# A gated recurrence and an expert layer in three-pass FP32: tokens per step from 512 to 468

## The reference

```python
# x, f_logit: (2, 6080, 256); w_in: (256, 2048); w_out: (2048, 256)
sig = 1 / (1 + exp(-f_logit))
f = lower_bound + (1 - lower_bound) * sig
i = 1 - f
for t in range(6080):
    h = f[:, t] * h + i[:, t] * x[:, t]     # one state per batch and channel
    y[:, t] = h
h = y.reshape(12160, 256) @ w_in
g = h * clip(h + 3, 0, 6) / 6
out = g @ w_out
```

## Time and profile before

| | |
|---|---|
| median of 3 runs | 1085.32 us (1084.63 to 1086.12) |
| span of the profiled execution, first to last instruction | 1083.2 us |
| around the span (median of the runs less the span) | 2.1 us |
| TensorE matmuls busy | 99% of the span, 4636 matmuls |
| VectorE / ScalarE / GpSimd busy | 57% / 49% / 7% |
| mean granted TensorE clock | 0.998 of full |
| memory traffic | 41.7 MB, 39 GB/s |

### The profile page before, as it was taken

The page is one execution under the profiler, slowest core; times in us unless marked ns, Lnnn a source line. Parts: engine busy times, 40 slices in busy tenths (PEclk is TensorE's granted clock), DMA queues, the critical chain, the costliest instruction groups (busy, mean ns, idle before and its releaser), DMA issues.

```text
span 1083.2 us, 12791 instructions
## 1 busy us (share of the span) xinstructions
PE 1074.5 (99%) x4636; PEld 873.8 (81%) x4636; DVE 621.4 (57%) x950; ACT 533.2 (49%) x859; POOL 70.9 (7%) x37
## 2 busy tenths in 40 slices
PE   7999999999999999999999999999999999999998
PEld 7998888888888888888888888888888888888886
DVE  7865564655646556465564655646556465564644
ACT  5655454454544545444454444544445445454443
POOL 3300000000000000000000000000000000000000
PEclk9999999999999999999999999999999999999999
DMA  7011010110101101011010110101101001010000
GB/s 262 1 56 56 1 59 0 58 58 0 58 6 52 58 0 58 13 46 58 0 58 17 41 58 0 58 21 37 58 0 58 24 34 58 0 58 20 1 20 19
DMA packets 22093, 41.74 MB, mean 39 GB/s; under 512 B 1600, under 2 KB 3136, under 8 KB 22080
## 3 DMA queue, kind: packets, MB, share of 16 engines
q1 hardware_dynamic: 22080, 41.56, 11.4%
HBM read 29.10 MB, written 12.45 MB: 38 GB/s over the span
## 4 chain that ended last, share of the span: by engine, by line
PE 98%; DVE 0%; ACT 0%; issue 0%; ACTq 0%
PE y_ps L465 49%; PE h_ps L445 49%; DVE state L349 0%; DVE state_lo L379 0%; ACT clipped L263 0%; DVE g_lo L364 0%; DVE g L359 0%; DVE drive L342 0%; ACT y_sb L324 0%; ACT state_hi L277 0%; ACT g_hi L268 0%; ACTq L262 0%
## 5 line engine op out<-in xcount | busy, mean ns | idle before, releaser
L263 ACT ACTIVATE clipped<-h_ps,half 128x512 f32<-128x512 f32 (+1 forms) x384 | 263.2, 686 | 533.6 <-PE h_ps L445 533.6
L359 DVE SCALAR_TENSOR_TENSOR g<-clipped,h_ps 128x512 f32<-128x512 f32 (+1 forms) x384 | 261.7, 682 | 450.2 <-ACT clipped L263 450.1
L445 PE MATMUL h_ps<-state_hi,w_in_hi 128*128 128x512 f32 (+1 forms) x768 | 303.2, 395 | 3.3 <-DVE state_lo L379 3.3
L465 PE MATMUL y_ps<-g_hi,w_out_hi 128*128 128x512 f32 (+1 forms) x768 | 302.5, 394 | 1.0 <-DVE g_lo L364 1.0
L445 PE MATMUL h_ps<-state_lo,w_in_hi 128*128 128x512 f32 (+1 forms) x768 | 302.8, 394 | 0.0
L445 PE MATMUL h_ps<-state_hi,w_in_lo 128*128 128x512 f32 (+1 forms) x768 | 302.7, 394 | 0.0
L465 PE MATMUL y_ps<-g_lo,w_out_hi 128*128 128x512 f32 (+1 forms) x768 | 302.3, 394 | 0.0
L465 PE MATMUL y_ps<-g_hi,w_out_lo 128*128 128x512 f32 (+1 forms) x768 | 302.3, 394 | 0.0
L364 DVE TENSOR_TENSOR g_lo<-g,g_hi 128x512 fp32r<-128x512 f32 (+1 forms) x384 | 271.2, 706 | 0.2
L268 ACT CAST g_hi<-g 128x512 fp32r<-128x512 f32 (+1 forms) x384 | 233.0, 607 | 1.6 <-DVE g L359 1.4
L445 PEld LDWEIGHTS h_ps<-state_hi,w_in_hi 128*128 128x128 f32 x768 | 144.9, 189 | 37.0 <-DVE state_lo L379 2.9
(11 more groups left out here) (23 smaller groups left out, 77.9 us busy)
## 6 DMA issues: line engine op xcount, KB each, us to landing
z_sb<-in_z SPq DMA_DIRECT2D x22, 512.0 KB, 4.5
x_sb<-in_x SPq DMA_DIRECT2D x22, 512.0 KB, 5.1
out_y<-y_sb SPq DMA_DIRECT2D x21, 512.0 KB, 3.3
w_in_raw<-in_w_in SPq DMA_DIRECT2D x8, 256.0 KB, 5.9
w_out_raw<-in_w_out SPq DMA_DIRECT2D x8, 256.0 KB, 7.1
out_y<-y_sb SPq DMA_DIRECT2D x2, 448.0 KB, 3.5
out_y<-y_sb SPq DMA_DIRECT2D x2, 256.0 KB, 2.1
z_sb<-in_z SPq DMA_DIRECT2D x2, 224.0 KB, 3.7
```

What stands on the lines that cost most here:

```text
L263: nc.scalar.activation(clipped[:, s, 0:n], h_ps[:, s, 0:n], ACT.Relu, bias=half[:], scale=1.0 / 6.0).then_inc(clipped_ready, 1)
L359: nc.vector.scalar_tensor_tensor(g[:, s, 0:n], clipped[:, s, 0:n], 1.0, h_ps[:, s, 0:n], ALU.min, ALU.mult).then_inc(g_ready, 1)
L445: last = nc.tensor.matmul(h_ps[:, s, 0:n], w[:, f, k, :], v[:, b, k, 0:n], start=(k == 0 and m == 0), stop=(k == K - 1 and m == len(terms) ...
L465: last = nc.tensor.matmul(y_ps[:, b, d, 0:n], w[:, f, at], v[:, s, 0:n], start=(f == 0 and m == 0), stop=(f == F - 1 and m == len(terms) - 1))
```

## The change

A step covers N = 468 tokens rather than 512. By the same formulas there are 13 steps (STEPS), the first of N_FIRST = 6080 - 12 x 468 = 464 tokens, and 26 tiles. Every tensor in SBUF with N in its shape gets rows of 468 elements (1872 bytes) rather than 512 (2048 bytes); the PSUM tensors keep rows of 512, one bank. The last copy on VectorE gets its range written out, since `y_ps` rows are now longer than N.

```diff
-N = 512
+N = 468
...
-            nc.vector.tensor_copy(y_sb[:, B - 1, 0], y_ps[:, B - 1, 0]).then_inc(y_head_copied, 1)
+            nc.vector.tensor_copy(y_sb[:, B - 1, 0, 0:N], y_ps[:, B - 1, 0, 0:N]).then_inc(y_head_copied, 1)
```

## The result

The changed kernel takes 1079.07 us (1078.64 to 1079.21, 4 runs) against 1085.14 us (1084.63 to 1086.12, 4 runs): ratio 0.9939, 95% interval 0.9926 to 0.9951. It is faster by 0.6%, 6.1 us. 15.3 us (1.4%) were forecast: the direction was right, and the gain is 40% of the forecast one.

The account below looks back on a forecast made before the run. The prediction took TensorE's matmul stream to bound the kernel: 18.1 start-up + 75.1 + 970.9 stream + 3.3 tail + 0.5 remainder = 1067.9 us of span, plus 2.1 around it, 1070.0 us; range 1057 to 1097.

Parts of the forecast that it names:

- What bounds the kernel, the counts, the other engines: Whole span: TensorE's matmul distance sets the time; 4608 and 360 matmuls after start-up; the other engines' work stays hidden.
- Start-up and tail: Before the first `down` matmul, 17.8 us growing by 0.3 to 18.1; after the last matmul, 3.3 us unchanged.
- the remainder of 0.5 us: Part of the earlier kernel's span that its account left unexplained (1082.7 against 1083.2), kept in the forecast sum.
- The time around the span: Measured time outside the profiled span, put at 2.1 us and added to 1067.9 us.
- The disputed price: Start-to-start distance of the new matmuls: 210.7 ns for 468 columns, 208.6 for 464, a stream of 1046.0 us.
- the point of decision: Distance of 213.8 ns a matmul, from which the stream has no more room for a gain.
- a distance outside 208 to 216 ns: Sign in the middle of the run that would make the step from the two sizes wrong.
- its last rival: Rows of 1872 bytes or an engine falling behind: up to 234.3 ns for each matmul, time 1188; chance 0.05.
- the line: Distance of the stream's matmuls interpolated between 448 and 512 columns: 15.6 us less stream, time 1070.0; chance 0.30.
- The flat addition: Stream matmuls keep 13.3 ns on top of the columns up to 468, rising only nearer 512: time 1058.4; chance 0.27.
- The snap to 213.3 ns: Both new sizes' distance goes to 16 units of 13.33 ns: time 1083.8, no change; chance 0.13, shared with near-decision cases.
- The fixed 21 ns: Each matmul pays 21 ns on top of its columns, 448 columns being the exception: time 1096.5, slower; chance 0.25.

Follow-up runs that it names:

- alone: Kernel cut down to TensorE stretches of 96 matmuls, recurrence and expert layer left out; 512 columns took 226.7 ns at shift 0, 234.3 at 40.
- ten different beginnings: TensorE-only stretches of 448 columns (rows of 448, shift 40), all but the first after one matmul of another size; all ten had 200.0 ns.
- the first sweep: TensorE-only kernel, 20 stretches of 96 matmuls of varied column counts, rows of 512 elements: 226.7 ns at 512 columns, 211.8 at 468, 202.6 at 448.

## Why the prediction was wrong

**What bounds the kernel, the counts, the other engines.** Right. TensorE is 98% of the chain, there are 4608 and 360 matmuls, no wait in the middle, slack 3.0 us as worked out, VectorE 59%, the loop's further turn and the further transfers cost nothing.

**Start-up and tail.** 18.1 was forecast and 17.6 measured; 3.3 and 3.3; the remainder of 0.5 us was not there. Together 1.0 us less. The trace before shows where the remainder was: the first 132 matmuls of the stream, from 17.80 to 44.64 us, took 0.44 us more than at 200.0 ns each. The time around the span was 1.9 us and not 2.1.

**The disputed price.** This step failed: "I take the straight line between the two rows", 210.7 ns for 468 columns and 208.6 for 464, with nothing for the new row length. Measured were 212.8 and 210.5: 4608 x 2.08 = 9.6 us and 360 x 1.9 = 0.7 us too little. Less the 1.0 and 0.2 us above, that is the miss of 9.1 us. Its direction held, since 212.8 lies below the point of decision, 213.8. The sign that was to show a wrong step here, "a distance outside 208 to 216 ns", was too wide to show it.

The fault was to take the distance for a function of the number of columns. The additions of 21.0 ns at 512 and 13.3 at 448 belong to the one place that both had in the kernel before. The same 512 columns have 13.3 ns when the states and g are moved by 352 bytes (1053.74 us), and the same 448 have 20.0 ns in a kernel of 448 tokens, even at their old place. What the runs show is a cost that depends on where the moving operand starts against the weights, in the main modulo 256 bytes, together with the size and, at 468 columns, with the steady pattern that the stream falls into.

**The row length.** The change also took the rows from 2048 to 1872 bytes. The prediction had this in its last rival, with a chance of 0.05, the price of 512 columns, and "No row speaks for it". The mechanism was there and its size was wrong: 2.8 ns a matmul, 12.2 us, not 118. Its ground was wrong as well: starts "at multiples of 2048 bytes", which the expectation for rows of 512 elements repeats, were starts 2048 bytes apart but 160 bytes off the weights' place. With rows kept at 512 elements the change gives 1066.91 us and 210.0 ns, near the line's 1070.0 and 210.7, so the missing gain went there: 2.8 ns more by the rows, 0.7 less than the line without them. That the line was near in this case is luck: the 464 columns took 212.2 ns there and not 208.6, and at the other place, 352 bytes on, the line's end points and its sign are different.

**The rivals.** The flat addition did not come: 13.3 ns was no floor for 468 columns in any run (15.0 was the least). The snap to 213.3 ns was near to what came, with 212.8, and its time of 1083.8 is 4.7 us too much; but alone, 468 columns do sit at 210.0, 211.7 or 213.3 by place and start. The fixed 21 ns was wrong in its premise, as shown by the kernel with 512 tokens at 13.3.

**Open.** Why the difference of the places counts is not shown. That the reads of the weights and of the moving operand get in each other's way would fit the 512 columns (both moved: no cost; bfloat16: 2.5 ns), but it is argued, and it does not by itself account for the other sizes: 448 columns are cheaper at 40 (200.0 ns) than at 0 (202.6), and 384, 496 and 504 have the same distance at both. The Trainium skill, "TensorE: Matmul & The Clock Gate", section "Part 2: What happens when you issue a matmul", says that loading the next weights takes nothing from the running matmul's reads. For FP32R the place of the weights does change the distance, 226.7 against 234.3 ns with nothing else changed; whether the reads are what it changes, no run here shows. Open is also whether the row length or the places behind it make the 2.8 ns, and why 448 columns have 206.7 ns in the whole kernel and 200.0 alone; ten different beginnings did not bring 206.7 about.

## What to carry to other kernels

When matmuls set the time, read the distance of their starts and subtract columns / 2.4; if what is left differs between stretches, ask about places in memory as well as sizes. A line through two sizes of one trace holds, if at all, for the addresses of that trace: before it is used for a change that moves them, one size should be measured at other addresses. A tensor's row length and whatever is allocated ahead of it belong to the change, though no instruction shows them; 352 unused bytes were worth 31 to 32 us here, five times what the change brought.

## What the runs showed of the hardware

- FP32R matmuls with a weight load each, back to back at the granted clock of 1.00 (2.4 GHz): 13.3 ns on top of the columns at 256 and 512 columns when moving operand and weights start at the same place modulo 256 bytes, up to 21.1 at 512 otherwise; 16 bytes of shift make 5.0 ns. bfloat16: 2.5 to 2.6 ns.
- At 512 columns the cost repeats with 64 elements of shift (256 bytes) in four pairs of five: 0 and 64, 16 and 80, 40 and 104, 56 and 120 agree to 0.1 ns; 32 and 96 differ by 0.8.
- The same place is not best for every size. Alone, with the moving operand 0 and 40 elements past the weights' place, in ns: 384 columns 173.3 to 173.6 and 173.3; 448 columns 202.6 and 200.0; 504 columns 226.7 to 226.9 and 226.7; 512 columns 226.7 and 234.3.
- 468 columns at one place had two steady distances, 210.0 and 213.3 ns, by what ran before.
- In the first sweep 504 columns took as long as 512 (226.9 and 226.7 ns), and 488 longer than 496 (225.6 and 223.3).
- Before the clock rose, at 0.50 (1.2 GHz), 448 columns had next to nothing on top of 373.3 ns.
